# Moving one rounding copy from VectorE to ScalarE, one step later, in the mish stage of an attention and two-MLP kernel

## What is computed

```python
x = attention(q, k, v, sigmoid(f_logit))            # 3072 tokens x 384
h = x @ w_in                                        # 384 -> 2048
sp = np.where(h > 20.0, h, np.log1p(np.exp(np.minimum(h, 20.0))))
x = (h * np.tanh(sp)) @ w_out                       # mish, 2048 -> 384
gate = 1 / (1 + np.exp(-(x @ w_gate)))              # 384 -> 1536
out = (gate * (x @ w_val)) @ w_out2                 # 1536 -> 384
```

## Time and profile before

| what | us |
|---|---|
| median of three runs | 1062.49 |
| the profiled execution | 1061.41 |
| its span in the trace | 1059.6 |
| PE busy | 1015.9 (96%) |
| DVE busy | 598.9 (57%) |
| ACT busy | 499.2 (47%) |
| POOL busy | 126.2 (12%) |
| share of PE in the chain that ended last | 80% |

### The profile page before, as it was taken

The page is one execution under the profiler, slowest core; times in us unless marked ns, Lnnn a source line. Parts: engine busy times, 40 slices in busy tenths (PEclk is TensorE's granted clock), DMA queues, the critical chain, the costliest instruction groups (busy, mean ns, idle before and its releaser), DMA issues.

```text
span 1059.6 us, 14103 instructions
## 1 busy us (share of the span) xinstructions
PE 1015.9 (96%) x4765; PEld 825.5 (78%) x4765; DVE 598.9 (57%) x939; ACT 499.2 (47%) x873; POOL 126.2 (12%) x147
## 2 busy tenths in 40 slices
PE   4999999799999999999999999999999999999997
PEld 3777777688887788877888788888888888888885
DVE  7999998677777777779999822222222222222221
ACT  5676776466667666676666512121312121312212
POOL 2212212500000000004444420000000000000000
PEclk9999999899999999999999999999999999999999
DMA  5444442200000000001111100000100000100001
GB/s 149 143 142 126 136 141 80 60 1 1 1 1 1 1 0 0 0 0 45 45 45 45 52 15 1 1 1 1 60 0 0 0 0 0 60 0 1 1 1 61
DMA packets 35344, 37.58 MB, mean 35 GB/s; under 512 B 4064, under 2 KB 26080, under 8 KB 35296
## 3 DMA queue, kind: packets, MB, share of 16 engines
q1 hardware_dynamic: 35296, 36.98, 11.7%
HBM read 32.24 MB, written 4.72 MB: 35 GB/s over the span
## 4 chain that ended last, share of the span: by engine, by line
PE 80%; DVE 10%; issue 6%; ACT 3%; DVEq 1%; DMA 0%; SPq 0%; ACTq 0%
PE bank L840 26%; PE bank L842 26%; PE bank L841 25%; DVE prefix L571 2%; DVE probs L598 1%; ACT qt L412 1%; PE bank L760 1%; PE bank L783 1%; DVE state L615 1%; DVE xlo L720 1%; DVE suffix L573 1%; DVE state L609 1%; PE bank L778 1%; DVE xlo L622 1%; DVE kb L587 1%
## 5 line engine op out<-in xcount | busy, mean ns | idle before, releaser
L840 PE MATMUL bank<-xhi,whi 128*128 (+1 forms) x720 | 285.3, 396 | 4.2 <-DVE xlo L720 2.6
L842 PE MATMUL bank<-xhi,wlo 128*128 (+1 forms) x720 | 283.8, 394 | 0.0
L841 PE MATMUL bank<-xlo,whi 128*128 (+1 forms) x720 | 281.4, 391 | 0.0
L740 DVE TENSOR_TENSOR prod<-prod,bank 128x512 f32<-128x512 f32 x72 | 49.5, 687 | 292.0 <-PE bank L842 292.0
L840 PE MATMUL bank<-ghi,whi 128*128 128x512 f32 x504 | 200.2, 397 | 8.2 <-DVE xlo L720 4.2
L842 PE MATMUL bank<-ghi,wlo 128*128 128x512 f32 x504 | 198.4, 394 | 0.0
L841 PE MATMUL bank<-glo,whi 128*128 128x512 f32 x504 | 197.0, 391 | 0.0
L840 PEld LDWEIGHTS bank<-xhi,whi 128*128 128x128 f32 x720 | 135.8, 189 | 33.8 <-DVE xlo L720 3.0
L842 PEld LDWEIGHTS bank<-xhi,wlo 128*128 128x128 f32 x720 | 135.6, 188 | 32.4
L841 PEld LDWEIGHTS bank<-xlo,whi 128*128 128x128 f32 x720 | 135.8, 189 | 31.0
L516 ACT ACTIVATE prod<-bank 128x512 f32<-128x512 f32 x72 | 43.2, 600 | 189.1 <-PE bank L842 189.1
(11 more groups left out here) (70 smaller groups left out, 1051.3 us busy)
## 6 DMA issues: line engine op xcount, KB each, us to landing
raw<-w_out_dram SPq DMA_DIRECT2D x28, 192.0 KB, 2.4
xb<-f_dram SPq DMA_DIRECT2D x48, 96.0 KB, 2.4
kb<-k_dram SPq DMA_DIRECT2D x48, 96.0 KB, 2.1
qb<-q_dram SPq DMA_DIRECT2D x48, 96.0 KB, 2.2
vb<-v_dram SPq DMA_DIRECT2D x24, 192.0 KB, 2.4
out_dram<-rows_out SPq DMA_DIRECT2D x18, 256.0 KB, 2.2
raw<-w_in_dram SPq DMA_DIRECT2D x16, 192.0 KB, 2.8
raw<-w_gate_dram SPq DMA_DIRECT2D x12, 192.0 KB, 2.5
```

The costliest lines, as they stand in the source:

```text
L740: dve.tensor_tensor(prod[:, i % NSET], prod[:, i % NSET], h_ps[1][:, :], ALU.mult).then_inc(p_done, 1)
L840: pe.matmul(ps, hi, xh, start=first, stop=False)
L841: pe.matmul(ps, hi, xl, start=False, stop=False)
L842: return pe.matmul(ps, lo, xh, start=False, stop=last)
```

## The change

The rounding copy to `ghi` is made by ACT instead of DVE, and both halves move one position later. ACT gets a function `high`, called with lag 1 between `start` and `angle`: at position i it rounds g of step i-1. DVE's `halves_of_g` becomes `low`, which only subtracts; it is called with lag 1 too, between `silu` and `cubic`. The waits for `g_done` and `acc_done` go with the copy to ACT. PE, POOL and SP are unchanged.

```diff
@@ ACT
+            def high(p, i):
+                act.wait_ge(g_done, p * N1 + i + 1)
+                wait(act, acc_done, p * N1 + i - 1)
+                act.activation(ghi[:, i % 2], sets[:, i % NSET, 1], ACT.Copy).then_inc(ghi_done, 1)
...
-                for lag, do in ((0, start), (0, angle), (0, square), (0, shifted)):
+                for lag, do in ((0, start), (1, high), (0, angle), (0, square), (0, shifted)):
@@ DVE
-            def halves_of_g(p, i):
-
-                dve.wait_ge(g_done, p * N1 + i + 1)
-                wait(dve, acc_done, p * N1 + i - 1)
-                dve.tensor_copy(ghi[:, i % 2], sets[:, i % NSET, 1]).then_inc(ghi_done, 1)
+            def low(p, i):
                 dve.wait_ge(ghi_done, p * N1 + i + 1)
                 dve.tensor_tensor(glo[:, i % 2], sets[:, i % NSET, 1], ghi[:, i % 2].bitcast(F32),
                                   ALU.subtract).then_inc(g_ready, 1)
...
-                for lag, do in ((0, silu), (0, cubic), (0, finish), (0, halves_of_g)):
+                for lag, do in ((0, silu), (1, low), (0, cubic), (0, finish)):
```

## The result

| | before | after |
|---|---|---|
| median of the runs, us | 1062.62 | 1086.32 |
| lowest to highest, us | 1061.41 to 1062.98 | 1085.74 to 1086.52 |
| span of the profiled execution, us | 1059.6 | 1083.0 |
| busy PE / DVE / ACT, us | 1015.9 / 598.9 / 499.2 | 1028.8 / 551.1 / 539.8 |

Each column holds four runs. The changed kernel is slower: the ratio is 1.0224, with a 95% interval of 1.0206 to 1.0242. That is 23.7 us, where 27 were forecast.

A forecast was written before the change was run, and what follows sets the result against it. PE, busy 96% of the span, bounds the kernel before; after, a 4.33 us ring outlasts its 4.15 us step. Terms 4.9 + 5.2 + 5.0 + 12 + 0.2 = 27.3 us give 1089.5 us, range 1075 to 1103.

The forecast's parts named there:

- The ring: Mish stage: copy, angle, square, shifted, cubic, finish, next copy take 4.33 us a turn against PE's step of 4.15.
- The one link that no row had shown: On ACT, from start of high(i) to start of angle(i+1): 0.54 us, bounds 0.48 and 0.67.
- First pass: First mish pass: high(31) starts at 333.1, where the replaced cast was at 328.23, late by 4.9 us.
- changes of pass: Mish stage, from last copy of one pass to that of the next: 5.2 and 5.0 us more.
- PE's waits at a change of pass: PE would wait about 1.9 us for low'(0) in place of its 1.45 us for xlo.
- the clock at nothing: Behind PE's waits at changes of pass: clock stays at 1.00, as after the 1.45 us wait, no cost.
- POOL: Last mish pass: POOL's weight splitting lengthens cubic by 0.80 us per pair of steps, 15 pairs, 12 us.
- the signs given: Last pass, for POOL: cubic at 1.3 to 1.5 us every second step, a pair of 9.4 to 9.5 us.
- Rival A: Last mish pass: ring is 4.33 us but POOL and DVE miss each other; +15.3, 1077 us; chance 0.18.
- Rival C: Mish stage: the ring closes within PE's 4.15 us, so not slower, 1062 us; chance 0.07.

The follow-up runs named there:

- experiment 1: Changed kernel with ACT's copy one place further down, between angle and square: 1060.31 us, ratio 0.9981 to the kernel before.
- experiment 2: Changed kernel with copy on ACT and subtraction on DVE in the same step, each last in its row: 1141.60 us, ratio 1.0749 to the kernel before.
- experiment 6: Changed kernel with POOL splitting only one column of each weight unit in the last mish pass: 1077.21 us, ratio 1.0141 to the kernel before.
- experiment 4: Changed kernel with ACT's copy at the end of its row, behind shifted: 1089.27 us, ratio 1.0266 to the kernel before.

## Why the prediction was right

- **The ring.** Forecast 4.33 us, measured 4.31; link by link the rows above differ from the terms by at most 0.02 us. The one link that no row had shown, the copy followed by an independent instruction, was taken as 0.54 and is 0.54.
- **That the ring, and not ACT's load, decides:** shown by experiments 1 and 2, which keep the instructions and change their order.
- **First pass and changes of pass:** 4.6 and 4.7 us for 4.9 and 5.2. In pass 2 nearly all of the difference is that of a turn of 4.32 to one of 4.33 over 30 turns. In pass 1 the small difference is partly luck, since three terms were off and cancelled: the first copy starts at 198.11 in place of 198.60, the first turn takes 5.29 us in place of 4.63, because POOL held cubic (1.05 us) and finish (1.32 us) up by 1.0 us and not by 0.3, and the other 30 turns take 0.5 us less.
- **PE's waits at a change of pass:** forecast 1.9 us, and 1.9 is the longest wait for glo at both. The clock stayed at 1.00 in the ring, as assumed. But the forecast also put the clock at nothing behind these waits, from a wait of 1.45 us that was followed by 1.00, and that held only at the first change of pass. At the second it cost 1.2 us.
- **POOL.** The place was right: low, then cubic, are the instructions hit, once per pair. The size was not: 0.80 us a pair was taken from a collision of before, and 0.50 is measured in 14 pairs (9.13 against 8.63) and 0.97 in the first. POOL starts 3.89 us after the copy (3.9 in the forecast), but its first cast ends 0.1 and its second 0.3 us sooner than I had reckoned, so cubic runs into a later part of the subtraction. Of the signs given, cubic at 1.3 to 1.5 us and a pair of 9.4 to 9.5 us were missed: they are 1.20 and 9.13. Twelve us were forecast for this term, and 8.0 are measured and shown to be POOL's by experiment 6. This is the mis-sized term; the 1.2 us of clock, which the sum left out, hide part of it in the total.
- **Rival A** (POOL misses DVE, 1077) is the kernel of experiment 6: 1077.2. It needed POOL's work to be cut away. **Rival C** is excluded by the measured 4.31.
- In the last pass cubic (1.20 us) and low (1.31 us) are still longer while POOL works, though DVE's cast is gone; in experiment 6, without POOL's work, both are back at a mean of 692 ns. The Trainium skill (SBUF — State Buffer, section "SBUF: two separate sides") has the rule that VectorE instructions with two SBUF inputs take the shared ports too, against a GpSimd instruction that reads SBUF, and not only those in a 2-port mode. The trace agrees.

What the prediction did not see is the second ring, through PE: it looked at whether `g_ready` comes late only by way of g. In the changed kernel that ring is open (the way from h to project is shorter, since the copy stands ahead of angle); it closes in experiment 4.

## What to carry to other kernels

When work moves between engines that run in written order, sum the ring, not the load: start at the waiting instruction, go through everything queued behind it that its successor needs, and come back; compare that with the period of the bounding engine. Here the same instruction cost 24 us, nothing, nothing and 27 us at four neighbouring places of one row. And ask for each delay that was hidden so far (here POOL's) whether its instruction lies on the new ring.

## What the runs showed of the hardware

- An activation copy of 128 x 512 from SBUF lasts 0.63 us, but an independent instruction starts 0.54 us after it; a dependent one of the other engine 0.65 to 0.67 us after its start (255.16 to 255.70 after the change; 254.36 to 255.01 in experiment 4; the earlier trace rows).
- PE can wait some 0.17 us in every 4.3 and be reported busy all the time, 20.00 of 20 us; the time of the weight loads (15.45 us against 16.32) and the count over 100 us (419 against 435) show it.
- What the clock does after a wait of PE can't be told from the length of the wait alone, not even within one execution. In the changed kernel a wait of 1.90 us at the first change of pass was followed by 1.00 and one of 1.92 us at the second by 0.57, with the same instructions ahead of both. Before, the 3.46 us wait was followed by 0.50. In the profile of experiment 1 a wait of 2.75 us at the same place was followed by 0.51, and a wait of 2.61 us at the start of the third stage by 1.00.
